# The token product of a fused attention and mixing kernel, turned to channel by token, with three token tiles per pass

## The reference, cut to what matters

```
attn = softmax(banded scores + bias) @ v          # window of 96 keys and 8 global keys
x    = attn, heads side by side                   # [2, 768, 512]
theta = x @ w_theta                               # 512 x 512, the angle stage
zr, zi = x * cos(theta), x * sin(theta)
y = w_tok_r @ zr + w_tok_i @ zi                   # 768 x 768 over tokens, the token product
u = x + y
v = u + relu(u @ w_ch)                            # 512 x 512, the channel product
h = relu(v @ w_in);  out = (h * sigmoid(conv3(h))) @ w_out
```

## Time and profile before

| | |
|---|---|
| median of 3 runs | 378.23 us |
| profiled execution, its own time | 378.37 us |
| its span, first to last instruction | 376.6 us |
| granted TensorE clock | 1.000 of full |
| PE busy / share of the chain that ended last | 371.8 us / 98% |
| DVE, ACT, POOL busy | 279.7, 220.5, 169.2 us |
| DMA read and written | 32.16 MB, 11.40 MB |

### The profile page before, as it was taken

One profiled execution on the slowest core, in us unless ns is written; L12 is line 12 of the kernel. 1 busy time (PEld: TensorE's weight loads), 2 busy tenths in 40 slices (PEclk: granted clock), 3 DMA queues, 4 the chain that ended last, 5 costly groups with the idle time before them and its releaser, 6 DMA issues.

```text
span 376.6 us, 6125 instructions
## 1 busy us (share of the span) xinstructions
PE 371.8 (99%) x2166; PEld 328.6 (87%) x2166; DVE 279.7 (74%) x639; ACT 220.5 (59%) x399; POOL 169.2 (45%) x137
## 2 busy tenths in 40 slices
PE   8999999999999999999999999999999999999996
PEld 3799999998888888888899889889888889999996
DVE  5686867765888799999797864346646966989782
ACT  3686868775776786442545274354577759945030
POOL 4999999998335300400000044100089926335720
DMA  6999889606200344323131243000600000002122
GB/s 201 409 415 379 299 322 312 242 21 270 8 0 3 112 150 186 106 103 85 42 85 42 77 125 106 3 0 1 224 1 0 2 0 0 3 0 85 42 101 110
DMA packets 15760, 43.98 MB, mean 117 GB/s; under 512 B 4464, under 2 KB 5744, under 8 KB 15728
## 3 DMA queue, kind: packets, MB, share of 16 engines
q1 hardware_dynamic: 15728, 43.57, 32.5%
HBM read 32.16 MB, written 11.40 MB: 116 GB/s over the span
## 4 chain that ended last, share of the span: by engine, by line
PE 98%; DVE 1%; issue 0%
PE bank L636 35%; PE bank L798 20%; PE bank L872 15%; PE bank L686 10%; PE bank L669 6%; PE bank L655 5%; PE bank L778 3%; PE bank L697 1%; PE bank L811 1%; PE bank L757 1%; DVE biased L1370 0%; DVE acc L1790 0%; DVE idle L1318 0%; DVE small L1384 0%; DVE small L1379 0%
## 5 line engine op out<-in xcount | busy, mean ns | idle before, releaser
L798 PE MATMUL bank<-b_ops,a_ops 128*128 128x512 f32 x324 | 75.5, 391 | 0.0
L798 PEld LDWEIGHTS bank<-b_ops,a_ops 128*128 128x128 f32 x324 | 60.5, 188 | 12.3
L636 PE MATMUL bank<-v_span,win 128*128 128x512 f32 x288 | 66.4, 390 | 0.0
L636 PEld LDWEIGHTS bank<-v_span,win 128*128 128x128 f32 x288 | 53.9, 188 | 11.0
L572 POOL TENSOR_TENSOR win<-winraw,win 128x1024 fp32r<-128x1024 f32 x4 | 9.6, 2402 | 69.7 <-ACT win L1078 69.7
L872 PE MATMUL bank<-bop,a_place 128*128 128x384 f32 x160 | 40.6, 334 | 0.0
L947 ACT ACTIVATE pT<-bank 128x512 f32<-128x512 f32 (+1 forms) x48 | 26.8, 558 | 18.5 <-PE bank L686 17.5
L636 PE MATMUL bank<-wth,xT 128*128 128x512 f32 x144 | 35.9, 399 | 0.0
L636 PE MATMUL bank<-uT,wch 128*128 128x384 f32 x192 | 34.8, 336 | 0.0
L636 PEld LDWEIGHTS bank<-uT,wch 128*128 128x128 f32 x192 | 33.7, 188 | 0.6
L686 PE MATMUL bank<-v_sb,pT 128*128 128x65 f32 x264 | 33.6, 268 | 0.0
(11 more groups left out here) (128 smaller groups left out, 751.1 us busy)
## 6 DMA issues: line engine op xcount, KB each, us to landing
qk_sb<-qk_laid SPq DMA_DIRECT2D x7, 792.0 KB, 10.3
w_raw<-w_tok_laid SPq DMA_DIRECT2D x6, 768.0 KB, 10.9
a_kept<-stage SPq DMA_DIRECT2D x6, 768.0 KB, 4.9
a_ops<-a_kept SPq DMA_DIRECT2D x6, 768.0 KB, 5.3
v_sb<-v_laid SPq DMA_DIRECT2D x5, 780.0 KB, 7.7
a_kept<-stage SPq DMA_DIRECT2D x9, 384.0 KB, 3.6
a_ops<-a_kept SPq DMA_DIRECT2D x9, 384.0 KB, 3.1
out<-acc SPq DMA_DIRECT2D x6, 384.0 KB, 2.3
```

The source lines that it names most:

```text
L636: last = pe.matmul(dst, w[a], m[b], start=(i == 0 and j == 0), stop=(i == n - 1 and j == 2))
L798: last = pe.matmul(y_bank(s)[:], a_ops[:, slot, hi, blk, :], b_ops[:, side, blk, lo, :], start=(blk == 0 and j == 0), stop=(blk == NT - 1 ...
```

## The change

The roles in the token product are swapped: `b_ops` (128 channels) is stationary and `a_ops` (three token tiles, 384 columns) moves, so that the result is channel by token. One step `mix_tokens(k, j)` makes 128 channels by 384 tokens of product k with 18 matmuls; there are 28 steps. The sums are no longer kept in x but in four arrays `yT`, which start as x turned: ACT copies each turned tile of the angle stage (`raw_x`), SP stores it to DRAM in pieces of 128 tokens per channel row, and loads it back by chunk (`load_y`), where x has been. `transpose_u` and the copy `u_raw` are gone; `high_u` reads `yT`. The split operands of three tiles are now released and loaded together. Some arrays have other places, one operand of the last stage has its two parts swapped, and the written orders of PE, ACT and DVE are new.

```diff
@@ SP
+            for t in range(TT):
+                sp.wait_ge(x_raw, t + 1)
+                sp.dma_start(x_kept_in[t // NI][:, :, t % NI, :], x_turned[:, t % 4]).then_inc(x_kept[t % 4], 16)
+
+            def load_y(chunk):
+                for n in range(4):
+                    sp.wait_ge(x_kept[n], 16 * (TT // 4))
+                sp.wait_ge(zf_ready, NT if chunk % 2 else TT)
+                sp.dma_start(yT[chunk][:], x_kept_in[chunk].rearrange("p j i c -> p j (i c)")).then_inc(y_in[chunk], 16)
@@ load_a
-                sp.wait_ge(y_ready, n + 1 if n < 4 else n + 3)
+                k, i = 2 + n // NI, n % NI
+                slot = a_slot(k, i)
+                sp.wait_ge(y_ready, CB * (k - 1))
...
-            for n in range(NA):
+            load_y(1)
+            load_y(3)
+            for n in range(NI):
+                load_a(n)
+            load_y(0)
+            load_y(2)
+            for n in range(NI, NA):
                 load_a(n)
@@ PE, x_tile
                 if t >= 2:
                     pe.wait_ge(x_lo, t - 1)
+                    pe.wait_ge(x_raw, t - 1)
@@ PE, token product
+            def turn(k, j, blk):
+                cols, first = slice(P * j, P * j + P), a_slot(k, 0)
+                for n, (hi, lo) in enumerate(((0, 0), (0, 1), (1, 0))):
+                    last = pe.matmul(y_bank(CB * k + j)[:, 0:HALF].rearrange("p (i c) -> p i c", i=NI),
+                                     b_ops[:, b_side(k), blk, hi, cols], a_ops[:, first:first + NI, lo, blk, :],
+                                     start=(blk == 0 and n == 0), stop=(blk == NT - 1 and n == 2))
+                if blk == NT - 1:
+                    last.then_inc(y_ready, 1)
...
-            def transpose_u(q, blks=range(CB)):
-                if blks[0] == 0:
-                    pe.wait_ge(u_ready, U_DONE[q])
...
-                for blk in blks:
-                    for i in range(NI):
-                        last = pe.transpose(u_bank(q)[blk][:, i * P:(i + 1) * P],
-                                            x[:, NI * MIXED[q] + i, blk * P:(blk + 1) * P], ident[:])
-                    last.then_inc(ut_ready, 1)
@@ ACT
+            def raw_x(t):
+                if t == 0:
+                    act.wait_ge(max_ready, 2 * NU)
+                act.wait_ge(x_lo, t + 1)
+                if t >= 4:
+                    act.wait_ge(x_kept[t % 4], 16 * (t // 4))
+                act.activation(x_turned[:, t % 4].rearrange("p c t -> p (c t)"), x_bank(t)[:], ACT.Copy).then_inc(x_raw, 1)
...
+            raw_x(0)
             for t in range(TT):
                 turns(t)
                 if t + 2 < TT:
                     high_x(t + 2)
+                if t + 1 < TT:
+                    raw_x(t + 1)
                 if t in TRIG_AT:
                     trigs(TRIG_AT[t])
@@ DVE
-            def add_y(s):
...
-                    last = dve.tensor_tensor(xt, xt, y_bank(s)[:], op)
+            def add_y(n):
+                k, j = divmod(n, CB)
...
+                    if j == 0 and k < 3:
+                        dve.wait_ge(y_in[chunk], 16)
+                    yt = yT[chunk][:, j, :]
+                    last = dve.tensor_tensor(yt, yt, y_bank(n)[:, 0:HALF], op)
@@ DVE, add_mix, for two of the first chunk's four parts
+                    dve.scalar_tensor_tensor(out=r, in0=r, scalar=0.0, in1=uT[:, j, :].bitcast(F32), op0=ALU.max,
+                                             op1=ALU.add).then_inc(v_step, 1)
+                    dve.wait_ge(v_step, j - 1)
+                    dve.tensor_tensor(r, r, u_low[:, j, :].bitcast(F32), ALU.add).then_inc(v_ready, 1)
```

More of the change, by code:

```diff
@@ L231, in s_bank, with y_bank, a_slot, low_of @@
             return psum[:, 2 * side:2 * side + 2, 256 * half:256 * half + 256]
[L233 to L234 removed]
+        def y_bank(n):
+            return bank[(4, 5, 0, 1, 6, 7)[n % 6]]
         def b_side(k):
             return (k + 1) % 2
[L239 to L243, removed]
+        def a_slot(k, i):
+            return NI * (k % 2) + i
+        def low_of(q, blk):
+            return u_low_first[blk][:] if q == 0 and blk < 2 else u_low[:, blk, :]
+        def b_part(k, part):
+            return 1 - part if k % 3 == 0 else part
         def pair(p):
@@ L775, in first_tokens @@
                     pe.wait_ge(z_lo, blk + 1)
-                    for i in range(NI):
[L777 to L793, removed]
+                    for j in range(CB):
+                        if blk == 0 and j == 2:
+                            pe.wait_ge(x_raw, TT)
+                        turn(0, j, blk)
@@ L794, in mix_tokens @@
+            def mix_tokens(k, j):
+                n = CB * k + j
+                if j == 0 and 2 <= k < 4:
+                    for i in range(NI):
+                        pe.wait_ge(a_in[a_slot(k, i)], 16 * (k // 2))
+                if j == 0 and k >= 4:
+                    pe.wait_ge(a_lo, NI * (k - 3))
+                if n >= 6:
+                    pe.wait_ge(u_ready, n - 5)
                 for blk in range(NT):
-                    if k >= 1 and i == 0 and blk % 2 == 0:
+                    if j == 0 and blk % 2 == 0:
@@ L796, in mix_tokens @@
                         pe.wait_ge(b_lo, NI * (k - 1) + blk // 2 + 1)
[L797 to L800, removed]
-            def transpose_u(q, blks=range(CB)):
-                if blks[0] == 0:
-                    pe.wait_ge(u_ready, U_DONE[q])
[L805 to L808, removed]
-                for blk in blks:
-                    for i in range(NI):
-                        last = pe.transpose(u_bank(q)[blk][:, i * P:(i + 1) * P],
-                                            x[:, NI * MIXED[q] + i, blk * P:(blk + 1) * P], ident[:])
-                    last.then_inc(ut_ready, 1)
+                    turn(k, j, blk)
@@ L824, in mix_channels @@
                 product(R_BANK[n % 2][:, 0:HALF], [([wch[:, part, blk, j * P:(j + 1) * P] for part in range(2)],
-                                                    [uT[:, part, blk, :] for part in range(2)])
+                                                    [uT[:, blk, :], low_of(q, blk)])
                                                    for blk in range(CB)], mix_ready)
@@ L1029, in high_b @@
                 if k >= 2 and two == 0:
-                    act.wait_ge(y_ready, NI * (k - 1))
+                    act.wait_ge(y_ready, CB * (k - 1))
                 if k == 1:
                     act.wait_ge(d_ready, two + 1)
+                    if two == 0:
+                        for n in range(4):
+                            act.wait_ge(x_kept[n], 16 * (TT // 4))
                 if k == 2:
@@ L1599, in _ @@
             own_difference(0)
+            weigh(7)
             own_difference(1)
@@ L1603, in _ @@
             low_b(1, 1)
-            weigh(7)
             low_b(1, 2)
@@ L1628, in _ @@
             low_b(3, 2)
-            add_mix(0)
-            add_y(8)
-            add_mix(1)
             sum_six(1)
             sum_six(2)
-            low_v(0)
-            add_y(9)
             sum_one(0)
             sum_one(1)
+            add_y(9)
+            low_b(4, 0)
+            add_mix(0)
+            sum_one(2)
+            low_v(0)
+            add_mix(1)
+            add_y(10)
+            low_a(7)
             low_v(1)
-            sum_one(2)
-            low_b(4, 0)
-            add_y(10)
-            add_y(11)
             low_a(6)
+            low_a(8)
             low_b(4, 1)
             low_b(4, 2)
+            add_y(11)
+            add_y(12)
+            add_y(13)
             add_mix(2)
             add_mix(3)
-            low_a(7)
             low_v(2)
+            add_y(14)
+            add_y(15)
+            low_u(1)
             low_v(3)
-            low_u(1)
-            add_y(12)
             sum_seven(0)
-            low_a(8)
             sum_seven(1)
@@ L1657, in _ @@
             add_mix(4)
+            low_a(10)
+            low_v(4)
             add_mix(5)
-            low_v(4)
-            add_y(13)
+            low_a(9)
+            low_v(5)
+            low_a(11)
             low_b(5, 0)
-            low_v(5)
-            low_a(9)
-            low_a(10)
             low_b(5, 1)
             low_b(5, 2)
-            add_y(14)
-            low_a(11)
+            add_y(16)
+            add_y(17)
+            add_y(18)
+            add_mix(6)
+            add_mix(7)
+            low_b(6, 0)
+            low_a(13)
             low_a(12)
-            low_b(6, 0)
-            add_y(15)
-            add_y(16)
+            low_a(14)
             low_b(6, 1)
             low_b(6, 2)
-            add_mix(6)
-            add_mix(7)
+            add_y(19)
+            add_y(20)
             low_v(6)
-            low_a(13)
-            add_y(17)
-            low_a(14)
+            add_y(21)
+            add_y(22)
+            add_y(23)
             low_u(2)
@@ L1683, in _ @@
             add_mix(8)
-            add_y(18)
+            add_mix(9)
             low_v(8)
-            add_mix(9)
```

213 lines of the change are left out of this document (114 added, 99 removed).

## The result

The changed kernel takes 374.86 us, the median of 6 runs (374.67 to 375.65), against 378.35 (378.17 to 378.90, 6 runs) before: a ratio of 0.9909, 95% interval 0.9899 to 0.9919. It is 3.5 us faster; 375.2 us was predicted, and the range was 374.3 to 377.0. The spans of the profiled executions are 373.1 and 376.6 us, at a granted clock of 0.999 and 1.000.

A forecast was written before the change was run, and what follows sets the result against it. PE was taken to bound the kernel, passing changes on one for one. Turns -5.2, token product +1.7, angle stage +0.3 and DVE +0.1 sum to -3.1 us: 375.2 us forecast, range 374.3 to 377.0.

The forecast's parts named there:

- The bound: From 112 to 260 us the chain holds only PE, so changes to its list move the end one for one.
- The turns: All 48 turns on PE, 109 ns each, are on the chain with nothing hiding them; removing them gives -5.2 us.
- The token product: On PE, 504 matmuls of 384 columns at 174 ns replace 378 of 512: 87.7 us against 86.0, +1.7.
- The angle stage: ACT's extra copy delays sine, `weigh` and `low_x`; PE waits 0.3 us in the last tile, bounds 0 and 1.2.
- The stores and loads: Stores of x land before `raw_x(4)` needs the place, and loads land during product 1: hidden, no cost.
- DVE in the token stage: DVE's parts of z for product 5 are ready with 0.1 to 0.3 us to spare; +0.1, bounds 0 and 1.5.
- The sum: Whole kernel: -5.2 + 1.7 + 0.3 + 0.1 = -3.1 us, median 375.2 us; the terms' bounds leave 374.5 to 376.0.
- (A): Rival: DVE cannot follow, with waits at product 5 and in the angle stage; 376.5 us, 377.5 at most; 12%.
- (B): Rival: in the angle stage ACT waits for a late store of x to free its place; 382 us; 6%.
- (C): Rival: the narrow token matmul costs more than 174 ns; a loss from 180 ns, 389 us at 202 ns; 4%.

The follow-up runs named there:

- e1: The changed kernel with 48 turns of 128 columns put back on PE, into columns that nothing reads: 380.12 us.
- e7: The kernel before with one turn for each column block instead of three, 32 turns fewer: 375.31 us.
- e9: The changed kernel with each token matmul of 384 columns made as three of 128 with the same stationary operand: 456.18 us, one run.
- e2: The changed kernel with sine and cosine of the fifth z tile taken in tile 9 of the angle stage instead of tile 8: 374.29 us.
- e3: The changed kernel with two places instead of four for the copies of the turned x: 379.08 us.
- e8: The changed kernel with each token matmul of 384 columns made as two of 256 with the same stationary operand: 408.34 us, one run.

## Why the prediction was right, step by step

**The bound.** PE alone, and each part passed on one for one: shown by e1, and by e7 up to 0.2 us of 3.5, which a wait for DVE took back.

**The turns.** -5.2 predicted, 5.24 on the chain before, 5.24 again in e1.

**The token product.** +1.7 predicted (87.7), +1.5 measured (87.5): 173.5 ns and not the 174 that I chose between the two rows. Three separate runs in the moving operand cost nothing, as the two runs in the expansion had suggested. By the estimate worked out from the rule that I weighed against the rows (the Trainium skill, "TensorE: Matmul & The Clock Gate", "Back-to-back issue gap") this part would have been +8.1 us. The trace disagrees: its 131 ns at 512 columns stand against 227 here, its 81 at 128 against 111 in e9.

**The angle stage.** +0.3 predicted in the last tile, +0.37 measured, by the path that the prediction named, and e2 removes it. The bound of 1.2 for the tiles with a turn ahead was not touched: their pieces are 2.77 and 0.44 throughout.

**The stores and loads.** Nothing was predicted and nothing was seen; the first landing fell at 98.8, in the 98.5 to 100.8 given.

**DVE in the token stage.** The size was near (+0.1 predicted; the four steps of the second chunk took 8.55 against 8.38, +0.17, while the others took 4.16 for 4.18), but the place was wrong, so that the size was near by luck. I looked at product 5's parts of z and gave them 0.1 to 0.3 to spare. No wait is named there, and at most 0.1 us can be: the piece of 108 matmuls took 18.81 us, and one and a half pieces of 12.48 are 18.72. What was late is `low_v(4)`, which the third channel step waits for, because a `low_a` stood between it and `add_mix(4)`. The count began at the end of the second step and so left that one out.

**The sum.** -5.24 + 1.47 + 0.37 + 0.06 for the channel steps (25.13 to 25.19 in all) = -3.3; the chain's last product ends at 370.25 instead of 373.66, -3.4, the span is 3.5 shorter, and the median too. The remaining 0.1 to 0.2 is not assigned, and it is no more than two executions of one kernel differ by. Of the 0.3 by which the prediction was too high, 0.2 is the matmul's price. One figure of the prediction does not follow from its terms: their own upper bounds give 375.2 + 0.3 + 0.9 + 1.4 = 377.8 and not 376.0. The range that it gave went to 377.0, and the measured time is in its lower part, so nothing hangs on it.

**The rivals.** (A) did not occur: the waits came to 0.5 to 0.6 us. (B) is real, and e3 shows its price; four places keep it off by 2.3 us. (C) would have begun at 180 ns.

## What to carry to other kernels

When one engine carries the whole chain, write a change as a sum of its instructions at prices read from the same trace, and only then look for the engine that is late. Swapping the operands of a product to save a turn pays here because the turns' 5.2 us exceed the narrower matmuls' 1.5. The width decides: at 256 columns the same work would be 756 matmuls at e8's 119.9 ns, 90.6 us or 4.6 more than before, and nearly nothing of the 5.2 would be left (an estimate from these prices, not run); at 128, as e9 shows, it is a heavy loss. When a copy is put on a side engine that has idle time, look for what stands behind it in the list, not at the idle time: both waits that this change brought (0.37 and 0.17 us) went away by moving a few calls in the lists, with no less work. Only the first came from the copy; the second came from the new order on DVE.

## What was not expected of the hardware

A matmul of 128 columns with its own load took 111 ns on average in this product (e9). Before, a turn took 109 and a matmul of 65 columns 105, so half the columns saved next to nothing, while from 256 columns on the price is 14 ns and 0.416 ns per column: 119.9 at 256, 173.5 at 384, 227 at 512. The busy time of the loads does not tell how near the floor is: in the changed kernel it fills the stretch (42.18 of 42.18 us) at 173.5 ns per matmul, while in e9 a load and a matmul follow every 111 ns. A full row of loads is no sign of being bound by them.
